# Second expert layer rebuilt: routing tile by tile beside the dense layer, a place table from one-hot matmuls, rows gathered per tile, two raw weight buffers

## The reference

```python
# 1. bucketed attention, B=2, H=8, S=768, D=64  ->  x of N=1536 rows, DM=512 columns
# 2. dense expert layer, E=8, FF=1024: every row goes through every expert
for e in range(E):
    out += P[:, e:e + 1] * (np.maximum(x @ w1[e], 0.0) @ w2[e])     # P from 8 Sinkhorn steps
# 3. second expert layer: every row goes through one expert
xn = x / (np.linalg.norm(x, axis=-1, keepdims=True) + 1e-06)
en = expert_emb / (np.linalg.norm(expert_emb, axis=-1, keepdims=True) + 1e-06)
logits = xn @ en.T / tau
expert_idx = np.argmax(logits, axis=1)
probs = np.exp(logits - logits.max(-1, keepdims=True)); probs /= probs.sum(-1, keepdims=True) + 1e-09
gate_w = probs[np.arange(N), expert_idx]
for e in range(E):
    mask = expert_idx == e
    out[mask] = gate_w[mask, None] * (np.maximum(x[mask] @ w1[e], 0.0) @ w2[e])
```

## Time and profile before

| | |
|---|---|
| median of 3 runs | 1652.41 us |
| profiled execution, its own time | 1649.05 us |
| its span, first to last instruction | 1647.3 us |
| PE busy | 1569.6 us, 95% |
| PEld, DVE, ACT, POOL busy | 80%, 37%, 29%, 20% |
| granted TensorE clock, mean | 0.978 of full speed |
| DMA, mean over the span | 70 GB/s |
| chain that ended last | PE 85%, DVE 4%, DMA 3%, issue 3%, POOL 3% |

### The profile page before, as it was taken

One profiled execution on the slowest core, in us unless ns is written; L12 is line 12 of the kernel. 1 busy time (PEld: TensorE's weight loads), 2 busy tenths in 40 slices (PEclk: granted clock), 3 DMA queues, 4 the chain that ended last, 5 costly groups with the idle time before them and its releaser, 6 DMA issues.

```text
span 1647.3 us, 21247 instructions
## 1 busy us (share of the span) xinstructions
PE 1569.6 (95%) x7516; PEld 1309.9 (80%) x7517; DVE 609.7 (37%) x1021; ACT 469.7 (29%) x864; POOL 324.4 (20%) x527
## 2 busy tenths in 40 slices
PE   7999999999999999999999999999999992799998
PEld 6899998788888888888888888888888771577776
DVE  5888888342221211211211322322222234554324
ACT  4777777112111111111111211211111132654113
POOL 4445444100300300210020030030030004332202
PEclk8999999999999999999999999999999995899999
DMA  4665664100100110110110110020020014754310
GB/s 121 177 156 141 157 141 162 52 1 0 69 35 1 62 40 0 51 51 0 51 51 0 51 51 0 0 102 0 0 82 21 0 52 141 262 191 143 132 45 24
DMA packets 50405, 115.94 MB, mean 70 GB/s; under 512 B 7862, under 2 KB 9910, under 8 KB 50368
## 3 DMA queue, kind: packets, MB, share of 16 engines
q1 hardware_dynamic: 44432, 102.39, 20.1%
q10 hardware_dynamic: 3536, 6.75, 1.5%
q0 software_dynamic: 2400, 6.31, 1.0%
HBM read 81.58 MB, written 13.40 MB: 58 GB/s over the span
## 4 chain that ended last, share of the span: by engine, by line
PE 85%; DVE 4%; DMA 3%; issue 3%; POOL 3%; ACT 1%; SPq 1%; DVEq 0%; ACTq 0%; POOLq 0%
PE psum L391 24%; PE psum L393 24%; PE psum L392 24%; PE psum L624 3%; DMA w_raw<-in_moe_w_dram 2%; PE psum L613 2%; PE psum L637 1%; PE psum L638 1%; PE psum L614 1%; PE psum L595 1%; PE psum L829 1%; DVE row_min L1118 1%; PE psum L649 1%; POOL x_sorted L530 1%; DVE pt_lo L1108 1%
## 5 line engine op out<-in xcount | busy, mean ns | idle before, releaser
L976 ACT ACTIVATE h_hi<-psum 128x512 fp32r<-128x512 f32 x192 | 114.9, 599 | 867.5 <-PE psum L393 867.5
L391 PE MATMUL psum<-xt_lo,w_hi 128*128 128x512 f32 x768 | 303.9, 396 | 0.2 <-DVE xt_lo L1213 0.2
L393 PE MATMUL psum<-xt_hi,w_lo 128*128 128x512 f32 x768 | 301.1, 392 | 0.0
L391 PE MATMUL psum<-w_lo,h_hi 128*128 128x512 f32 x768 | 300.0, 391 | 0.0
L393 PE MATMUL psum<-w_hi,h_lo 128*128 128x512 f32 x768 | 299.3, 390 | 0.0
L392 PE MATMUL psum<-w_hi,h_hi 128*128 128x512 f32 x768 | 298.9, 389 | 0.0
L392 PE MATMUL psum<-xt_hi,w_hi 128*128 128x512 f32 x768 | 298.8, 389 | 0.0
L1298 DVE SCALAR_TENSOR_TENSOR h_lo<-psum,h_hi 128x512 fp32r<-128x512 f32 x192 | 132.7, 691 | 360.8 <-ACT h_hi L976 360.7
L424 POOL CAST w_hi<-w_raw 128x512 fp32r<-128x512 f32 x64 | 39.9, 624 | 813.1 <-PE psum L393 803.8
L1341 DVE SCALAR_TENSOR_TENSOR tok<-psum,route,tok 128x512 f32<-128x512 f32 x84 | 57.5, 744 | 384.6 <-PE psum L393 384.6
L393 PEld LDWEIGHTS psum<-xt_hi,w_lo 128*128 128x128 f32 x768 | 144.2, 188 | 33.4
(11 more groups left out here) (236 smaller groups left out, 1903.5 us busy)
## 6 DMA issues: line engine op xcount, KB each, us to landing
w_raw<-in_moe_w_dram SPq DMA_DIRECT2D x32, 2048.0 KB, 8.3
k_hh<-k_hi SPq DMA_DIRECT2D x32, 192.0 KB, 3.0
x_sorted<-zeros SPq DMA_DIRECT2D x21, 257.0 KB, 3.9
x_row<-x_sorted ACTq DMA_DIRECT2D x19, 256.0 KB
k_raw<-in_k_dram SPq DMA_DIRECT2D x8, 384.0 KB, 3.2
v_raw<-in_v_dram SPq DMA_DIRECT2D x16, 192.0 KB, 3.5
k_b<-k_lo SPq DMA_DIRECT2D x16, 192.0 KB, 3.3
q_raw<-in_q_dram SPq DMA_DIRECT2D x7, 384.0 KB, 3.7
```

Source lines behind the costliest of these rows:

```text
L391: pe.matmul(acc, a[0], b[1], start=start, stop=False)
L393: return pe.matmul(acc, a[1], b[0], start=False, stop=stop)
L976: act.activation(h_s[0][:, f, :], psum[:, f % 4, :], ACT.Relu).then_inc(m1.h_hi, 1)
```

## The change

The second layer's preparation is rewritten.

- **Routing by row tile.** For each 128-row tile t of `tok`: PE turns it (`turn_token`), ACT copies it (`token`), PE multiplies it in plain float32 by the embeddings (`token_logits`), DVE picks the expert (`choose`), PE counts the rows of the same expert before each row (`token_rank`), DVE writes two one-hot matrices (`find_cell`), PE multiplies them (`table_part`), and DVE adds the product to a table (`add_part`) that holds for each place its row number. Tiles 0 to 3 run beside the downs of chunk 1 of the last dense expert (`tokens_beside`), 4 to 6 beside the ups of chunk 2, 7 to 10 beside its downs (`tokens_between`), 11 behind it.
- **Rows stay where they are.** SP stores each `tok` tile plainly to `x_rows` and later the weights to `weights`; POOL gathers 128 rows by number for each tile, and 128 weights (`gather`). The scatter, `x_sorted`, its clears and `meta` go, and so do ACT's row loads.
- **Weights.** The first two experts' `w1` have raw buffers of their own, `w2` has two raw buffers all along. POOL makes the first two `lo` parts of `w1` and every `lo` part of `w2`; DVE keeps `w1` from expert 2 on.
- `turn_h(i, 1)` moves from down step 2 to down step 1; 16 transposes with no use for the result stand before the first tile.

```diff
...
+        def store_x(t):
+            sp.wait_ge(m1.y, (E - 1) * TT + t + 2)
+            sp.dma_start(x_rows_v[t // IT, :, t % IT, :], tok[:, t, :]).then_inc(s_x_stored, 16)
+        for t in range(2 * CT):
+            store_x(t)
+        sp.wait_ge(m1.up, CH * KF * E + 1)
+        sp.wait_ge(m2.w1_in, 16)
+        sp.dma_start(w1_odd_raw[:], m2.wa[1]).then_inc(m2.w1_in, 16)
+        store_x(2 * CT)
         sp.wait_ge(m2.w1_lo, 1)
-        sp.dma_start(w1_raw[:], m2.wa[1]).then_inc(m2.w1_in, 16)
-
-        sp.wait_ge(s_sorted, 16 * TT)
-        sp.dma_start(meta[:, 1:, :], x_sorted[0:SLOTS * P, DM:ROW].rearrange("(i p) c -> p i c", p=P)).then_inc(s_meta, 16)
-        sp.wait_ge(m2.w2_lo, HF)
-        sp.wait_ge(s_w2_pool, KF - HF)
-        sp.wait_ge(s_xrow, 16)
-        sp.dma_start(w2_raw[:], m2.wb[1]).then_inc(m2.w2_in, 16)
-        with sp.Fori(2, E) as e:
-
+        sp.wait_ge(m2.w1_in, 32)
+        sp.dma_start(w1_raw[:], m2.wa[2]).then_inc(m2.w1_in, 16)
+        for t in range(2 * CT + 1, TT):
+            store_x(t)
+        sp.wait_ge(s_x_stored, 16 * TT)
+        sp.wait_ge(s_squares, 2 * CT)
+        sp.wait_ge(m2.w2_in, 16)
+        sp.dma_start(w2_odd_raw[:], m2.wb[1]).then_inc(m2.w2_in, 16)
+        sp.wait_ge(s_p_ready, 1)
+        sp.dma_start(weights_v, per_tok[:, 2, :].rearrange("p (b t) -> p b t", b=B)).then_inc(s_p_stored, 16)
+        sp.wait_ge(m2.w2_lo, KF)
+        sp.wait_ge(m2.w2_in, 32)
+        sp.dma_start(w2_raw[:], m2.wb[2]).then_inc(m2.w2_in, 16)
+        for e in range(3, E):
+            sp.wait_ge(m2.w2_lo, KF * (e - 1))
+            sp.wait_ge(m2.w2_in, 16 * e)
+            sp.dma_start(w2_raw_p[e % 2][:], m2.wb[e]).then_inc(m2.w2_in, 16)
             sp.wait_ge(m2.w1_lo, e)
+            sp.wait_ge(m2.w1_in, 16 * e)
             sp.dma_start(w1_raw[:], m2.wa[e]).then_inc(m2.w1_in, 16)
...
+        def first_w1_lo(e, u, raw):
+            for kd in range(KD):
+                pool.wait_ge(m2.w1_hi, KD * e + kd + 1)
+                ins = pool.tensor_tensor(w1_p[u][1][:, kd, :], raw[:, kd, :], w1_p[u][0][:, kd, :].bitcast(F32),
+                                         ALU.subtract)
+            ins.then_inc(m2.w1_lo, 1)
+        def w2_lo2(e, u, raw, fs=range(KF)):
+            for f in fs:
                 pool.wait_ge(m2.w2_hi, KF * e + f + 1)
-                pool.tensor_tensor(w2_p[u][1][:, f, :], w2_raw[:, f, :], w2_p[u][0][:, f, :].bitcast(F32),
-                                   ALU.subtract).then_inc(s_w2_pool, 1)
+                pool.tensor_tensor(w2_p[u][1][:, f, :], raw[:, f, :], w2_p[u][0][:, f, :].bitcast(F32),
+                                   ALU.subtract).then_inc(m2.w2_lo, 1)
+        def gather(dst, src, idx, done):
+            pool.indirect_dma_start(dst, None, src, bass.IndirectOffsetOnAxis(ap=idx, axis=0)).then_inc(done, 16)
...
         def store(i):
             pool.wait_ge(s_y2, i + 1)
-            copy(idx_now[:], out_idx[:, bass.ds(i, 1)]).then_inc(s_idx, 1)
+            pool.wait_ge(s_xrow, 16 * i + 32)
+            copy(idx_now[:], tab[:, bass.ds(i, 1), :].rearrange("p i c -> p (i c)")).then_inc(s_idx, 1)
             pool.wait_ge(s_idx, i + 1)
             pool.sem_inc(s_pool_go, 1)
-            pool.indirect_dma_start(out, bass.IndirectOffsetOnAxis(ap=idx_now[:], axis=0), y_row[:], None,
+            pool.indirect_dma_start(out, bass.IndirectOffsetOnAxis(ap=idx_now[:, 0:1], axis=0), y_row[:], None,
                                     bounds_check=N - 1, oob_is_err=False).then_inc(s_out2, 16)
-            pool.wait_ge(s_out2, 16 * i + 16)
-            pool.sem_inc(s_y_free, 1)
...
+                gather(p_now[:], weights, idx_now[:, 1:2], s_p)
+                pool.wait_ge(s_xrow_t, i + 2)
+                pool.sem_inc(s_pool_go, 1)
+                gather(x_row[:], x_rows, idx_now[:, 2:3], s_xrow)
+                pool.wait_ge(s_out2, 16 * i + 16)
+                pool.wait_ge(s_p, 16 * i + 16)
+                pool.sem_inc(s_y_free, 1)
+        first_w1_lo(0, 0, w1_raw)
+        first_w1_lo(1, 1, w1_odd_raw)
+        w2_lo2(0, 0, w2_raw, range(0, 2))
+        pool.wait_ge(s_x_stored, 16 * TT)
+        pool.wait_ge(s_first_idx, 1)
+        gather(x_row[:], x_rows, first_idx[:], s_xrow)
+        w2_lo2(0, 0, w2_raw, range(2, 5))
+        pool.wait_ge(m2.routed, 1)
+        pool.wait_ge(s_xrow_t, 1)
+        gather(x_row[:], x_rows, tab[:, 1, 1:2], s_xrow)
+        w2_lo2(0, 0, w2_raw, range(5, KF))
+        w2_lo2(1, 1, w2_odd_raw)
+        pool.wait_ge(s_p_stored, 16)
...
+        def turn_token(t, bank):
+            pe.wait_ge(m1.y, (E - 1) * TT + t + 2)
+            if t > 0:
+                pe.wait_ge(s_squares, t)
+            for kd in range(KD):
+                tr = pe.transpose(psum[:, bank, kd * P:kd * P + P], tok[:, t, kd * P:kd * P + P], ident[:])
+            tr.then_inc(s_turned, 1)
+        def token_logits(t, bank):
+            pe.wait_ge(s_copied, t + 1)
+            for kd in range(KD):
+                mm = pe.matmul(psum[:, bank, 0:E], x_t[:, kd, :], emb_t[:, kd, :], start=(kd == 0), stop=(kd == KD - 1))
+            mm.then_inc(s_logits, 1)
+        def token_rank(t, bank):
+            pe.wait_ge(s_chosen, t + 1)
+            pe.matmul(psum[:, bank, 0:E], prior[:], chosen[:], start=True, stop=False)
+            pe.matmul(psum[:, bank, 0:E], ones[:], counts[:, t % 2, :], start=False, stop=True).then_inc(s_rank, 1)
+        def table_part(t, bank):
+            pe.wait_ge(s_cell, t + 1)
+            if t > 0:
+                pe.wait_ge(s_added, t)
+            pe.matmul(psum[0:CELLS, bank, 0:P], cell[:].rearrange("p e r -> p (e r)"), lane_id[:], start=True,
+                      stop=True).then_inc(s_table, 1)
+        def tokens_beside(j, n):
...
+        def tokens_between(f, i, n):
+            t = 2 * CT - 1 + i
+            if f == 2:
+                turn_token(t, 0)
+            if f == (3 if i == 0 else 1):
+                if i == 0:
+                    pe.wait_ge(m1.h_lo, KF * n + 7 + 5)
+                table_part(t - 1, 3)
+            if f == 4:
+                token_logits(t, 1)
+            if f == 7:
+                token_rank(t, 2)
...
+        table_part(TT - 2, 3)
+        turn_token(TT - 1, 0)
+        token_logits(TT - 1, 1)
+        token_rank(TT - 1, 2)
+        pe.wait_ge(s_total_in, 1)
+        pe.matmul(psum[0:E, 5, 0:1], counts[:, TT % 2, :], ones[:, 0:1], start=True, stop=True).then_inc(s_total, 1)
+        table_part(TT - 1, 3)
+        pe.wait_ge(s_added, TT)
+        pe.matmul(psum[:, 4, 0:1], table[0:CELLS, :], ident[0:CELLS, 0:1], start=True, stop=True).then_inc(s_first, 1)
+        pe.wait_ge(s_begin_in, 1)
+        pe.matmul(psum[0:CELLS, 6, 32:33], earlier[0:E, :], spot[0:E, 5:6], start=True, stop=True)
+        pe.matmul(psum[0:1, 6, 48:48 + E + 1], spot[0:E, 4:5], reach[0:E, :], start=True, stop=True).then_inc(s_begin, 1)
+        pe.wait_ge(s_slot_in, 1)
+        pe.matmul(psum[:, 7, 0:COLS], table[0:CELLS, :], slot_of[0:CELLS, :], start=True, stop=True).then_inc(s_slots, 1)
+        for i in range(16):
+            pe.transpose(psum[:, 3, 0:P], ident[:], ident[:])
...
-                    if f == 2:
+                    if f == 1:
...
+        def token(t, bank):
+            if t > 0:
+                act.wait_ge(s_logits, t)
+            act.wait_ge(s_turned, t + 1)
+            act.copy(x_t[:].rearrange("p k i -> p (k i)"), psum[:, bank, :]).then_inc(s_copied, 1)
+            act.wait_ge(s_copied, t + 1)
+            act.activation(psum[:, bank, :], tok[:, t, :], ACT.Square,
+                           accum_out=per_tok[:, 0, t:t + 1]).then_inc(s_squares, 1)
...
+        def choose(t, bank):
+            dve.wait_ge(s_logits, t + 1)
+            scores_, best = psum[:, bank, 0:E], per_tok[:, 4, t:t + 1]
+            link(dve.tensor_reduce(best, scores_, AX.X, ALU.max))
+            link(dve.scalar_tensor_tensor(pick[:], scores_, best, per_exp[:, 3, :], ALU.is_ge, ALU.mult))
+            link(dve.tensor_reduce(spot[:, 0:1], pick[:], AX.X, ALU.max))
+            link(dve.tensor_scalar(chosen[:], pick[:], spot[:, 0:1], None, ALU.is_equal))
+            dve.sem_inc(s_chosen, 1)
+            link(dve.tensor_tensor(counts[:, (t + 1) % 2, :], counts[:, t % 2, :], chosen[:], ALU.add))
+            if t == TT - 1:
+                dve.sem_inc(s_total_in, 1)
+            link(dve.tensor_copy(logit[:, t, :], scores_))
+        def find_cell(t, bank):
+            dve.wait_ge(s_rank, t + 1)
+            link(dve.tensor_tensor(pick[:], psum[:, bank, 0:E], chosen[:], ALU.mult))
+            link(dve.tensor_reduce(spot[:, 1:2], pick[:], AX.X, ALU.add))
+            link(dve.tensor_scalar(spot[:, 2:3], spot[:, 1:2], -(P / 2 - 0.5), EVEN, ALU.add, ALU.add))
+            link(dve.scalar_tensor_tensor(spot[:, 3:4], spot[:, 2:3], EVEN, spot[:, 1:2], ALU.subtract, ALU.subtract))
+            link(dve.tensor_scalar(lane_id[:], lane[:], spot[:, 3:4], tok_id[:, t:t + 1], ALU.is_equal, ALU.mult))
```

(11 more changed lines are left out.)

441 lines of the change are left out of this document (223 added, 218 removed).

## The result

The changed kernel takes 1678.7 us (median of 4 runs, 1678.2 to 1679.6), the kernel before 1652.5 in the same session: ratio 1.0158, 95% interval 1.0141 to 1.0176. It is 26 us slower; the forecast was 22 us faster. Its profiled execution has a span of 1676.8 us, where the sum had 1625.2.

What follows compares the result with a forecast made beforehand. PE was taken to bound the last dense expert, with time to win in the gap and tiles behind; 19.9 - 24.8 - 10.3 - 6.4 - 0.5 = -22.1 took the span from 1647.3 to 1625.2 us, median 1630, range 1612 to 1648.

Steps and rivals of the forecast that it cites:

- Term 1: Last dense expert: 14.5 us of net added PE work, 1.5 of tight hand-overs, 3.9 of lock waits; +19.9 us.
- Rival B: Last dense expert: POOL's wide pieces hold DVE up in full, 19.5 us instead of 3.9; 1646 us, chance 0.15.
- Term 2: Gap between dense and second layer: 42.3 us becomes 17.5, by a counted routing chain and first gather; -24.8 us.
- D: Gap: the routing chain behind the dense layer is longer than counted, gap stays near 30; 1643 us, chance 0.10.
- Term 3: First five tiles of the second layer: weight loads leave the chain, POOL is late next; 86.3 becomes 76, -10.3 us.
- A cycle of 15.6: First five tiles: POOL's time per one-tile expert, 5.2 us for store and gathers plus 10.4 for subtractions, against PE's 12.7.
- C: First five tiles: POOL's cycle is 23.3 us through overlap with DVE's w1 and later gathers; 1657 us, chance 0.10.
- Term 4: Other twelve tiles: POOL catches up, DVE has fewer subtractions, so its relu is ready; 159.4 becomes 153, -6.4 us.
- Terms 5: Attention and tail: the 21 clears issued by SP go, -0.5 us, between 0 and -3; the tail stays the same.

Runs made afterwards that it cites:

- a3: The changed kernel with five small tensors (192 bytes) moved ahead of tok, so xt lies 192 bytes later and w1_hi where it was: 1669.8 us.
- b2: The kernel before with 192 unused bytes per partition ahead of w1_hi, nothing else: 1661.8 us, ratio to before 1.0050.
- c1: The changed kernel without POOL's eight 128x1024 subtractions for the first two experts' w1 (lo parts left out, PE's matmuls kept): 1670.4 us.
- k1: The changed kernel with small tensors ahead of tok, first w1 and half of later w2 subtractions on DVE, some POOL pieces later, x_lo(0) earlier: 1626.3 us.
- d1: The changed kernel with one more POOL wait: its last three pieces for expert 0 and eight for expert 1 start behind DVE's p_ready: 1679.6 us.
- j1: The changed kernel with turn_h(i, 1) back at down step 2: 1683.5 us.
- b1: The kernel before with turn_h(i, 1) one down step earlier and SP's wait for the cleared tile behind the next pair's loads: 1640.6 us, ratio 0.9936.
- a1: The changed kernel with 96 unused bytes per partition behind tok, shifting xt and all buffers behind it: 1680.5 us.
- a2: The changed kernel with 32 unused bytes per partition ahead of w1_hi alone: 1682.8 us.

## Why the prediction was wrong, step by step

- **Missed altogether: the dense layer.** I read the edits of `place` as bookkeeping, and the sum has no term for them. They cost 8 to 9 us (a3 9.0, b2 7.9, 8.9 by the chunks), 7.3 of them ahead of the last expert and 0.9 in it.
- **Term 1, its waits, is a step that failed.** The expert grew by 34.4 us, not 19.9. The added matmuls were 3.0 us more than the 14.5 forecast: c1's expert, without POOL's pieces, is 19.3 us longer than before, less 0.9 of placement and 0.9 of waits. For DVE behind POOL I had taken half a piece three times, 3.9. Seven operations were held, `spot`, `chosen` and `lane_id` among them, six of them for nearly a whole piece, 12.5 us in all, and PE waited 9.8 for it. And I priced no clock for a PE that waits: some 5.4 more. Rival B had the mechanism. That its 19.5 lies near the 15.2 is in part luck: it was for waits alone.
- **Term 2.** The gap shrank by 18.0, not 24.8. `slot_of` took 4.66 us behind three pieces, and behind it stood 16 transposes (3.5 us) that my chain did not have at all. The first gather was issued 12.7 us behind the last down, not 10.6: `chosen` took 1.0 more, and the logits 1.9 instead of 1.4 at a granted clock of 0.50. k1, where `slot_of` is quick, has 19.2. D's 30 was not reached.
- **Term 3 is the larger failure.** "A cycle of 15.6" was 21.0, 20.8 and 20.2. I took 5.2 for the store with its gathers, from a scatter that lands after 2.8 us in a quiet stretch; beside a weight load a gather takes 6 to 8, and copy, issues and waits come to 9.9. The 1.2 us for that contention stood in the gap, where the load had landed by the time the gather was issued (3.7 us to landing), and was left out of the cycle. The 22.8 us that the stage is longer than forecast are 4.9 at its start (POOL's first store at +18.4, not +13.5), 15.2 in three cycles and 2.7 behind the fourth store. The wait of 12.7 us in tile 0, which I had foreseen for no stage, is no further term: without it, in d1, the first store is as late and the five tiles take 101.0. C said 99.1, by a cycle of 23.3 and an overlap that came only in part (10.9 for the pieces, not 15.3), so its number is nearer than its sum. It had 0.10.
- **Term 4.** 153 came out as 152.9 for another reason: j1 shows that `turn_h` is the whole of it.
- **Terms 5.** The first dense relu comes 2.7 us earlier, not 0.5. b1 keeps the clears and has 1.9 of it, so it is mostly SP's wait for the cleared tile, with the next pair's loads behind it; the changed kernels' profiles differ among themselves by as much (280.9 to 283.6 us against 285.2 and 284.9), so the transfers' own share isn't shown. The tail is 2.4 longer. Only 0.2 of it lies ahead of the last store, which waits for a gather whose rows nobody uses; the other 2.1 lie behind the store's issue, where no engine is busy, and their cause stays open.
- **The chances.** B and C were taken as alternatives and held at once, since both come from the work given to POOL beside DVE and beside gathers. That k1's span of 1624.9 is the forecast's 1625.2 is luck in part: its stages are 156, 19, 77 and 151 against 158, 17.5, 76 and 153, but in k1 DVE does the first `w1` subtractions and half of the later `w2` ones, which the forecast had on POOL.

## What to carry to other kernels

Work moved to POOL is priced with what DVE has beside it, a whole piece of POOL for nearly every DVE operation in a chain that PE waits for (more may come, as the 12.8 us show), and with the lower clock behind a long wait; wide pieces go where DVE has no chain, or are cut short. A queue's cycle is summed from every issue and landing in it, with the transfers that it triggers itself still moving. An edit of the allocation is an edit of the time: compare the spacing of matmuls that the diff does not touch.

## What the runs showed of the hardware that was not expected

- A matmul with 512 moving float32 columns was issued every 0.229 or every 0.233 us in the dense ups, by the distance between the two operands' places in a partition. It was fast where `w1_hi` lies 448 bytes above a multiple of 2048 from `xt_hi` (before, a3, b1, k1) and slow at 640 (after, a1, b2) and 672 (a2); the downs, at 0, took 0.227 everywhere. In the second layer the weights are the moving operand. Counted the same way, from the moving operand to the stationary one, the ups and downs of its odd experts have 544 in before, 640 in after and 448 in a3 and k1, and those of the even ones 0. An odd tile took 0.2 us more than an even one in before and after, 0.004 for each of its 48 matmuls, and in k1 the difference is gone (12.33 and 12.30 us), as in a3. This fits, but no run moved these distances by themselves. The two distances that were fast, 0 and 448, are not enough for a rule: that the multiple is 2048, and not a smaller power of two, was not tried.
- A DVE operation of 0.17 us was held for 12.8 us, over eleven instructions of POOL, where others had to wait for one.
- DVE's and POOL's subtractions side by side (d1) were done in 13.97 us, from POOL's first to its last; alone they take 4.63 (DVE, in after at 1440.26) and 9.79, 14.4 in sum: next to nothing of it overlaps.
